# A sequence-mixing and MLP kernel: ScalarE issues the last piece's four stores of the first batch

## The chip, the cores and the metric

The kernel runs on one core of one Trainium2 chip. A core has TensorE (matmuls), VectorE, ScalarE, GpSimd and SyncE, and 16 DMA engines that all of them share. DMAs are issued from instruction queues, here from SyncE's and, for indirect ones, from GpSimd's. The metric is the device time of one execution in microseconds (us), lower is better.

## The reference

Three stages follow each other on x of shape (4, 4224, 192), batch by sequence by channels:

```python
# 1: causal convolution over the sequence, 7 taps per head, taps = softmax(weight), 8 heads of 24 channels
out = np.einsum('hk,bskhg->bshg', w, x_unf)
# 2: low-rank mixing over the sequence, then an MLP over the channels (192 -> 768 -> 192)
h = xt @ U @ V                        # U (4224, 32), V (32, 4224)
u = x + h.transpose(0, 2, 1)
x = u + np.maximum(u @ w_ch1, 0.0) @ w_ch2
# 3: real part of a 2D Fourier transform over sequence and channels, layer norm, an MLP
mixed = np.real(np.fft.fft(np.fft.fft(x, axis=1), axis=2))
u = x + mixed
un = (u - mean(u)) / np.sqrt(var(u) + 1e-06)
out = u + np.maximum(un @ w_ch1, 0.0) @ w_ch2
```

Stage 2 needs x @ U summed over the whole sequence of a batch (called t) before its first block can start. That is why the convolution of the first batch stands alone at the beginning.

## The kernel before

The program is written by hand, one instruction stream for each engine, with semaphores between them. fp32 operands are split in a high part and a low part in fp32r, and each product is made of several matmuls; hence the `..h`, `..l` and `..s` tiles.

**The opening.** The first batch is convolved in four pieces (`PIECES`, `NP` = 4) of 9, 9, 9 and 8 tiles of 122 rows, each in four pairs of heads (`PAIRS` = 4, so `FILLS` = 16 pairs in a batch). For each pair TensorE multiplies by the band matrix (line 910), ScalarE copies the result from the bank back into `xin0` (`first_convolved`, recorded as line 995, as all of ScalarE's copies are) and raises `act_x`. ScalarE and VectorE split the piece into `xhl`, and TensorE multiplies it by U (line 894) to add up t. After the last piece ScalarE copies the first V part (`v_high(0)`, `vch<-vraw`) and two pieces of the weights; VectorE makes their low parts and the sum of t (`tsb`, lines 1327 to 1331), both split it into `tst` (line 1355), and TensorE multiplies `tst` by V for the first block (`low_rank`, line 832).

**The convolved rows** go to HBM as well (`x_conv`), since the blocks of stage 2 read them in another layout. SyncE stores each piece (`store_x`) once its four pairs are copied: two stores of 112 and 10 rows (line 636), and for the last piece two more of 64 and 12 rows (line 640) for its last tile. When all stores of the batch have landed (`x_stored`, semaphores `x_out`, line 471), SyncE loads the first block into `ub` (`load_u`, line 659) and GpSimd the second, which is read backwards, with an indirect DMA (line 1498). VectorE adds the low-rank product to `ub` (line 1218 and 1221), TensorE transposes it (line 845), and the MLP begins (lines 792 to 815).

**The order on the queues.** SyncE's queue is in the order of the code: loads of x, U and V, the weights, the stores of the four pieces, the first `ub` load, the second weight of the MLP, the next batch's x, eight loads of V, then the stores and loads of V by way of `v_split`. V in split form goes out to HBM once and comes back block by block (`load_v`, lines 593 and 594), the first time for the third block.

**After the opening** 88 blocks of 384 rows follow (11 for each batch, and that twice, for stages 2 and 3). The convolution of later batches, the Fourier stages and the groups of spectrum rows are placed into numbered slots between the MLP matmuls.

Of the kernel before, what the change touches and what calls it, by code (L numbers as in the profile page):

```python
# [13 lines left out]
S, D, H, K, R = 4224, 192, 8, 7, 32  # L14
# [18 lines left out]
CT = N1 - PAD  # L33
NT = -(-S // CT)
TAIL = S - CT
OVER = (NT - 1) * CT - TAIL
PW = 9
PIECES = [(p, min(PW, NT - p)) for p in range(0, NT, PW)]
NP = len(PIECES)
PAIRS = H // 2  # L40
FILLS = NP * PAIRS
# [105 lines left out]
def program(nc, x, weight, U, V, w1a, w2a, w1b, w2b, f1, low, high, bc, mirror, backward_in, ident_in, out):  # L147
# [5 lines left out]
    xc = [hbm(f"x_conv{b}", (S, D)) for b in range(B)]  # L153
# [5 lines left out]
    with ExitStack() as ctx:  # L159
        def sb(name, shape, dt):  # L160
            return ctx.enter_context(nc.sbuf_tensor(name, shape, dt))

        def sem(name):
            return ctx.enter_context(nc.semaphore(name))
# [3 lines left out]
        with ExitStack() as early:  # L168
            xin0 = early.enter_context(nc.sbuf_tensor("xin0", [128, NT, D], F32))
# [5 lines left out]
        xin = [sb(f"xin{n + 1}", [128, PW, D], F32) for n in range(2)]  # L175
# [135 lines left out]
        for b in range(B):  # L311
            n0 = at[(0, b, 0)]
            for u in range(NB):
                w = b * NB + u
# [31 lines left out]
        for c in range(1, B):  # L346
# [13 lines left out]
            for k, (n, m) in enumerate(spots):  # L360
                p, first = k // 2, k % 2 * 2
# [67 lines left out]
        x_out = [sem(f"x_out{n}") for n in range(2)]  # L429
# [27 lines left out]
        def taken(e, key):  # L457

            q, k = fills[key]
            e.wait_ge(tb_free[q], k + 1)  # L460
# [3 lines left out]
        def pieces_out(c, p):  # L464

            return c * 64 + (p // 2 + 1) * 32 if p % 2 == 0 else c * 96 + (32 if p < NP - 1 else 96)

        def x_stored(e, c):

            e.wait_ge(x_out[0], pieces_out(c, NP - 2))  # L470
            e.wait_ge(x_out[1], pieces_out(c, NP - 1))

        def pair_of(c, p, k):

            return c * FILLS + p * PAIRS + k
# [72 lines left out]
        def _(e):  # L548
# [68 lines left out]
            def load_x(c, p):  # L617
                if c > 1 or p > 1:
                    before = (c, p - 2) if p > 1 else (c - 1, p + 2)
                    e.wait_ge(x_out[p % 2], pieces_out(*before))  # L620
                    e.wait_ge(pool_xl, pair_of(*before, PAIRS) - FILLS)
                j0, w = PIECES[p]
                e.dma_start(xin[p % 2][:, 0:w, :], x[c, :, j0:j0 + w, :]).then_inc(x_in[p % 2], 16)

            def store_x(c, p):
                j0, w = PIECES[p]
                src = xin0[0:CT, j0:j0 + w, :] if c == 0 else xin[p % 2][0:CT, 0:w, :]
                if c == 0:
                    e.wait_ge(act_x, pair_of(c, p, PAIRS))
                else:  # L630
                    taken(e, ("conv", c, p, PAIRS - 2))
                    taken(e, ("conv", c, p, PAIRS - 1))
                whole = w if p < NP - 1 else w - 1
                for a, z in ((0, 112), (112, CT)):
                    dst = bass.AP(xc[c].tensor, (j0 * CT + a) * D, [[D, z - a], [CT * D, whole], [1, D]])
                    e.dma_start(dst, src[a:z, 0:whole, :]).then_inc(x_out[p % 2], 16)
                if whole < w:
                    for a, z in ((OVER, OVER + 64), (OVER + 64, CT)):
                        dst = bass.AP(xc[c].tensor, (TAIL + a) * D, [[D, z - a], [1, D]])
                        e.dma_start(dst, src[a:z, whole, :]).then_inc(x_out[p % 2], 16)  # L640

            def rising(n, t):

# [7 lines left out]
            def load_u(n):  # L651
                if backward(n):
                    return
                ph, b, i = blocks[n]
                u_free(e, n)
                if i == 0:
                    x_stored(e, b)
                src, slot = rising(n, xc)
                e.dma_start(slot, src).then_inc(u_in[n % UR], 16)
# [44 lines left out]

            load_w1(0, w1a)
            store_x(0, 0)
            store_x(0, 1)
            store_x(0, 2)
            store_x(0, 3)
            load_u(0)  # L710
            load_w2(0, w2a)
            load_u(1)
# [58 lines left out]
            for t in range(TB):  # L771
                dst = bass.AP(out.tensor, b * (S * D) + (i * TB + t) * D, [[N2 * D, 128], [1, D]])
# [12 lines left out]
        def _(e):  # L785
# [92 lines left out]
            def part_of_t(c, p):  # L878
                j0, w = PIECES[p]
                if c == 0:  # L880
                    e.wait_ge(u_l, min(p + 1, len(U_PARTS)))
                    e.wait_ge(dve_xl, pair_of(0, p, PAIRS))
                    src = xhl if p % 2 == 0 else xhl1
                else:
                    e.wait_ge(pool_xl, pair_of(c, p, PAIRS) - FILLS)
                    src = xhl
                if c == 0:
                    q, first, last = 0, p == 0, p == NP - 1
                    o = tb[q]
                else:  # L890
                    o, q = empty(e, ("t", c, p))
                    first, last = True, True
                for j in range(w):
                    mm = e.matmul(o[0:2 * R, 0:2 * D], uhl[0:CT, j0 + j, :], src[0:CT, j].rearrange("p a d -> p (a d)"),  # L894
                                  start=(first and j == 0), stop=(last and j == w - 1))
                mm.then_inc(pe_tb[q] if last else pe_t0, 1)
# [96 lines left out]
        def _(e):  # L993
            def copy(o, i):
                return e.activation(o, i, ACT.Copy)  # L995
# [87 lines left out]
            def first_convolved(p, k):  # L1083
                f, j0 = pair_of(0, p, k), PIECES[p][0]
                bk = CONV_BANKS[f % len(CONV_BANKS)]
                e.wait_ge(pe_cv, f + 1)
                copy(tiles_of_pair(xin0[:, j0:], p, k), bank_of_pair(bk, p)).then_inc(act_x, 1)

            def first_high(p, k):
                wait(e, pe_t0, p - 1)  # L1090
                e.wait_ge(act_x, pair_of(0, p, k) + 1)
                copy(tiles_of_pair((xhl, xhl1)[p % 2][:, :, 0], p, k), tiles_of_pair(xin0[:, PIECES[p][0]:], p, k))\
                    .then_inc(act_xh, 1)

            def u_high(n):
                j = slice(*U_PARTS[n])
                e.wait_ge(ld_u, 16)
                copy(uhl[:, j, 0:R], u_raw[:, j]).then_inc(u_h, 1)
# [20 lines left out]
            def weights_high(n, part):  # L1119
                if part == 0:  # L1120
                    e.wait_ge(ld_w1[n], 48)
                    copy(w1h[n][:], w1l_raw[n][:]).then_inc(w_h[n], 1)
                elif part == 1:
                    copy(w1s[n][:], w1t_raw[n][:]).then_inc(w_h[n], 1)
                else:
                    e.wait_ge(ld_w2[n], 16)
                    copy(w2[n][:, :, 0:D], w2_raw[n][:, :, D:2 * D]).then_inc(w_h[n], 1)
# [3 lines left out]
            def v_high(n):  # L1131
                a, z = (v * 128 for v in V_PARTS[n])
                e.wait_ge(ld_v[n], 64)
                if n == 3:
                    e.wait_ge(v_stored[2], 16)
                copy(vpart[n], vraw[:, a:z]).then_inc(v_h, 1)

            for p in range(NP):
                for k in range(PAIRS):
                    first_convolved(p, k)  # L1140
                for k in range(0, PAIRS, 2):
                    first_high(p, k)
                if p < len(U_PARTS):
                    u_high(p)
            v_high(0)
            weights_high(0, 0)
            weights_high(0, 1)
# [425 lines left out]
```

## Time and profile before

| | |
|---|---|
| timed runs | 1247.24 us median of 3 (1245.2 to 1247.64) |
| the profiled execution | 1249.38 us, its span 1247.6 us |
| TensorE busy | 1217.3 us, 98% |
| VectorE busy | 829.9 us, 67% |
| ScalarE busy | 678.7 us, 54% |
| GpSimd busy | 424.3 us, 34% |
| SyncE's and GpSimd's queues | 133.95 MB and 18.99 MB |
| first transposes of TensorE (line 845) | from 37.47 us |

The span runs from the first to the last instruction of the profiled execution. Its own time is 1.8 us longer, and that execution is 2.1 us above the median of the timed ones. PE is TensorE, PEld its weight loads, DVE VectorE, ACT ScalarE, POOL GpSimd, SP SyncE; a q behind the name (SPq) is the engine's instruction queue, where DMAs are issued. L636 is line 636 of the kernel. An issue's duration is the time for which it held its queue; the data lands later.

### The profile page before, as it was taken

To read this page: it belongs to the slowest core of one execution; us is meant where nothing else is said; L and a number is where in the kernel's file an instruction comes from. 1 tells how busy PE (TensorE), PEld (TensorE's weight loads), DVE (VectorE), ACT (ScalarE), POOL (GpSimd) and SP (SyncE) were. 2 spreads that over 40 slices of the span, in tenths; PEclk is the share of its full clock that TensorE was granted. 3 is DMA by queue.
4 is the path that set the end of the run, shared out by engine and by line. 5 is a ranking of instruction groups with operands and counts; after the bars stand their busy time and mean duration, and the time that the engine had idled before them with its cause. 6 is when DMAs were issued, how large, how long until landed. Compare 5 with 4: busy or idle time off the path is not lost.

```text
span 1247.6 us, 23842 instructions
## 1 busy us (share of the span) xinstructions
PE 1217.3 (98%) x8404; PEld 1189.8 (95%) x8404; DVE 829.9 (67%) x2238; ACT 678.7 (54%) x1779; POOL 424.3 (34%) x541
## 2 busy tenths in 40 slices
PE   6899999999999999999999999999999999999998
PEld 5799999999998999999999999999999999999998
DVE  5565576777675577655556877765666777766564
ACT  5355555444566655445555666544445656655554
POOL 0133342343343245323333344521212344433331
PEclk9899999999999999999999999999999999999999
DMA  9867543344556533224434322322333233232221
GB/s 293 277 210 222 177 142 91 106 135 135 162 182 215 183 115 97 75 69 133 130 105 136 118 88 90 94 63 76 92 101 107 71 110 96 90 99 86 75 74 35
DMA packets 87967, 154.48 MB, mean 124 GB/s; under 512 B 11480, under 2 KB 47043, under 8 KB 87804
## 3 DMA queue, kind: packets, MB, share of 16 engines
q1 hardware_dynamic: 80232, 133.95, 34.0%
q0 software_dynamic: 7616, 18.99, 4.8%
q8 instruction: 68, 1.11, 0.4%
q14 instruction: 51, 0.42, 0.1%
HBM read 94.59 MB, written 63.32 MB: 127 GB/s over the span
## 4 chain that ended last, share of the span: by engine, by line
PE 93%; DMA 2%; DVE 2%; POOL 1%; SPq 1%; issue 1%; ACT 1%; ACTq 0%; POOLq 0%
PE bank L811 20%; PE bank L812 9%; PE bank L792 8%; PE bank L799 7%; PE bank L800 7%; PE bank L796 7%; PE bank L793 7%; PE bank L815 4%; PE bank L910 3%; PE bank L845 2%; PE bank L873 2%; PE bank L933 2%; PE bank L875 2%; PE bank L874 2%; PE bank L814 2%; PE bank L894 2%
## 5 line engine op out<-in xcount | busy, mean ns | idle before, releaser
L1005 ACT ACTIVATE ht<-bank 128x384 fp32r<-128x384 f32 x528 | 259.0, 491 | 472.0 <-PE bank L800 470.7
L1201 DVE SCALAR_TENSOR_TENSOR ht<-bank,ht 128x384 fp32r<-128x384 f32 x528 | 293.7, 557 | 332.7 <-ACT ht L1005 329.0
L811 PE MATMUL bank<-w,ht 128*128 128x384 f32 x1320 | 418.6, 366 | 0.8 <-DVE ub L1209 0.5
L812 PE MATMUL bank<-w,ht 128*128 128x192 f32 x1320 | 330.9, 251 | 0.0
L1460 POOL TENSOR_TENSOR ub<-ub,tmp 128x576 f32<-128x576 f32 x87 | 124.4, 1430 | 452.2 <-DVE ub L1209 310.6
L811 PEld LDWEIGHTS bank<-w,ht 128*128 128x128 f32 x1320 | 248.9, 189 | 3.9 <-issue 3.1
L812 PEld LDWEIGHTS bank<-w,ht 128*128 128x128 f32 x1320 | 252.4, 191 | 0.0
L792 PE MATMUL bank<-uth,w1h 128*128 128x384 f32 x528 | 189.4, 359 | 0.0
L799 PE MATMUL bank<-uts,w1s 128*128 128x384 f32 x528 | 179.0, 339 | 0.6 <-DVE uts L1234 0.6
L796 PE MATMUL bank<-utl,w1h 128*128 128x384 f32 x528 | 178.9, 339 | 0.5 <-DVE utl L1226 0.5
L793 PE MATMUL bank<-uth,w1l 128*128 128x384 f32 x528 | 178.8, 339 | 0.0
L800 PE MATMUL bank<-uts,w1t 128*128 128x384 f32 x528 | 178.2, 337 | 0.0
L1509 POOL DMA_INDIRECT mixed<-rowm,mir x84 | 82.7, 985 | 217.3 <-DVE rowm L1307 214.3
L793 PEld LDWEIGHTS bank<-uth,w1l 128*128 128x128 f32 x528 | 101.3, 192 | 0.0
L799 PEld LDWEIGHTS bank<-uts,w1s 128*128 128x128 f32 x528 | 99.5, 188 | 1.8 <-DVE uts L1234 1.4
L796 PEld LDWEIGHTS bank<-utl,w1h 128*128 128x128 f32 x528 | 99.8, 189 | 1.2 <-DVE utl L1226 1.2
L792 PEld LDWEIGHTS bank<-uth,w1h 128*128 128x128 f32 x528 | 100.1, 190 | 0.5 <-issue 0.5
L800 PEld LDWEIGHTS bank<-uts,w1t 128*128 128x128 f32 x528 | 99.5, 188 | 0.0
L815 PE MATMUL bank<-w,ht 128*128 128x384 f32 x264 | 81.9, 360 | 0.0
L1483 POOL TENSOR_TENSOR xhl<-xin,xhl 128x432 fp32r<-128x432 f32 (+1 forms) x48 | 52.4, 1113 | 82.3 <-ACT xhl L995 82.3
L873 PE MATMUL bank<-f1t,x2h 128*64 128x132 f32 (+1 forms) x264 | 62.6, 250 | 4.3 <-issue 3.7
L814 PE MATMUL bank<-w,ht 128*128 128x192 f32 x264 | 66.7, 253 | 0.0
(127 smaller groups left out, 2273.4 us busy)
## 6 DMA issues: line engine op xcount, KB each, us to landing
f1t<-f_copy SPq DMA_DIRECT2D x44, 396.0 KB, 3.3
ub<-x_two SPq DMA_DIRECT2D x44, 288.0 KB, 3.1
mix<-mixed SPq DMA_DIRECT2D x44, 288.0 KB, 3.3
out<-ub SPq DMA_DIRECT2D x43, 288.0 KB, 2.1
xin<-in_x SPq DMA_DIRECT2D x12, 864.0 KB, 7.1
x_conv<-xin SPq DMA_DIRECT2D x12, 756.0 KB
vch<-v_split SPq DMA_DIRECT2D x42, 192.0 KB, 2.8
mixed<-rowk SPq DMA_DIRECT2D x88, 74.2 KB
```

Of the source, the lines that this page charges most:

```text
L792: e.matmul(o, w1h[ph][:, c], uth[:, par], start=True, stop=False)
L793: e.matmul(o, w1l[ph][:, c], uth[:, par], start=False, stop=False)
L796: e.matmul(o, w1h[ph][:, c], utl[:, par], start=False, stop=False)
L799: e.matmul(o, w1s[ph][:, c], uts[:, par], start=False, stop=False)
L800: e.matmul(o, w1t[ph][:, c], uts[:, par], start=False, stop=True).then_inc(pe_up, 1)
L811: e.matmul(dn[t][:, 0:2 * D], hh, w2[ph][:, m, :], start=(m == 0), stop=False)
L812: mm = e.matmul(dn[t][:, 0:D], hl, w2[ph][:, m, 0:D], start=False, stop=False)
L814: e.matmul(dn[t][:, 0:D], hl, w2[ph][:, m, 0:D], start=False, stop=False)
L815: e.matmul(dn[t][:, 0:2 * D], hh, w2[ph][:, m, :], start=False, stop=True)\
L1005: e.activation(hth[q % 4], up[q % 3][:, 0:TOK], ACT.Relu).then_inc(act_h, 1)
L1201: e.scalar_tensor_tensor(htl[q % 4], up[q % 3][:, 0:TOK], 0.0, hth[q % 4].bitcast(F32), ALU.max, ALU.subtract).then_inc(dve_l, 1)
L1460: e.tensor_tensor(u_slot(n), u_slot(n), tmp[:], ALU.add).then_inc(pool_y, 1)
```

## The change

The stores of a piece become a function of their own, `piece_out`, that takes the engine which issues them. SyncE's `store_x` calls it after its wait, as before, for every piece but the last of the first batch. For that one ScalarE waits for `act_x` at 16 (all pairs copied) and calls `piece_out`, between its last `first_high` and `v_high(0)`. The semaphores that the stores raise, and the waits for them, are the same.

```diff
--- before.py
+++ after.py
@@ -470,6 +470,19 @@
             e.wait_ge(x_out[0], pieces_out(c, NP - 2))
             e.wait_ge(x_out[1], pieces_out(c, NP - 1))
 
+        def piece_out(e, c, p):
+
+            j0, w = PIECES[p]
+            src = xin0[0:CT, j0:j0 + w, :] if c == 0 else xin[p % 2][0:CT, 0:w, :]
+            whole = w if p < NP - 1 else w - 1
+            for a, z in ((0, 112), (112, CT)):
+                dst = bass.AP(xc[c].tensor, (j0 * CT + a) * D, [[D, z - a], [CT * D, whole], [1, D]])
+                e.dma_start(dst, src[a:z, 0:whole, :]).then_inc(x_out[p % 2], 16)
+            if whole < w:
+                for a, z in ((OVER, OVER + 64), (OVER + 64, CT)):
+                    dst = bass.AP(xc[c].tensor, (TAIL + a) * D, [[D, z - a], [1, D]])
+                    e.dma_start(dst, src[a:z, whole, :]).then_inc(x_out[p % 2], 16)
+
         def pair_of(c, p, k):
 
             return c * FILLS + p * PAIRS + k
@@ -623,21 +636,12 @@
                 e.dma_start(xin[p % 2][:, 0:w, :], x[c, :, j0:j0 + w, :]).then_inc(x_in[p % 2], 16)
 
             def store_x(c, p):
-                j0, w = PIECES[p]
-                src = xin0[0:CT, j0:j0 + w, :] if c == 0 else xin[p % 2][0:CT, 0:w, :]
                 if c == 0:
                     e.wait_ge(act_x, pair_of(c, p, PAIRS))
                 else:
                     taken(e, ("conv", c, p, PAIRS - 2))
                     taken(e, ("conv", c, p, PAIRS - 1))
-                whole = w if p < NP - 1 else w - 1
-                for a, z in ((0, 112), (112, CT)):
-                    dst = bass.AP(xc[c].tensor, (j0 * CT + a) * D, [[D, z - a], [CT * D, whole], [1, D]])
-                    e.dma_start(dst, src[a:z, 0:whole, :]).then_inc(x_out[p % 2], 16)
-                if whole < w:
-                    for a, z in ((OVER, OVER + 64), (OVER + 64, CT)):
-                        dst = bass.AP(xc[c].tensor, (TAIL + a) * D, [[D, z - a], [1, D]])
-                        e.dma_start(dst, src[a:z, whole, :]).then_inc(x_out[p % 2], 16)
+                piece_out(e, c, p)
 
             def rising(n, t):
 
@@ -706,7 +710,6 @@
             store_x(0, 0)
             store_x(0, 1)
             store_x(0, 2)
-            store_x(0, 3)
             load_u(0)
             load_w2(0, w2a)
             load_u(1)
@@ -1142,6 +1145,8 @@
                     first_high(p, k)
                 if p < len(U_PARTS):
                     u_high(p)
+            e.wait_ge(act_x, FILLS)
+            piece_out(e, 0, NP - 1)
             v_high(0)
             weights_high(0, 0)
             weights_high(0, 1)
```

On ScalarE, at the end of the opening, the order before was (`xin` and `xhl` are the last piece's copies, `vch` the first V part, `w1h` and `w1s` pieces of the first weight, `tst` the split sum t, `vmid` the second V part):

```order
L995 ACTIVATE xin<-bank 122x8x48 x4
L995 ACTIVATE xhl<-xin 122x8x48 x2
L995 ACTIVATE vch<-vraw 128x768
L995 ACTIVATE w1h<-w1l_raw 128x768
L995 ACTIVATE w1s<-w1t_raw 128x768
L995 ACTIVATE tst<-tsb 32x192 x2
L995 ACTIVATE vmid<-vraw 128x1152
```

and is now:

```order
L998 ACTIVATE xin<-bank 122x8x48 x4
L998 ACTIVATE xhl<-xin 122x8x48 x2
L480 DMA x_conv<-xin 112x7x192
L480 DMA x_conv<-xin 10x7x192
L484 DMA x_conv<-xin 64x192
L484 DMA x_conv<-xin 12x192
L998 ACTIVATE vch<-vraw 128x768
L998 ACTIVATE w1h<-w1l_raw 128x768
L998 ACTIVATE w1s<-w1t_raw 128x768
L998 ACTIVATE tst<-tsb 32x192 x2
L998 ACTIVATE vmid<-vraw 128x1152
```

Four DMA issues stand ahead of the first V copy and of all that ScalarE does later; nothing else has moved there.

On SyncE, from the third piece's stores, the order before was (`ub<-x_conv` is the first block's load, `w_raw` the second MLP weight):

```order
L636 DMA x_conv<-xin 112x9x192
L636 DMA x_conv<-xin 10x9x192
L636 DMA x_conv<-xin 112x7x192
L636 DMA x_conv<-xin 10x7x192
L640 DMA x_conv<-xin 64x192
L640 DMA x_conv<-xin 12x192
L659 DMA ub<-x_conv 128x576
L581 DMA w_raw<-in_moe_w_ch 128x6x192
```

and is now:

```order
L480 DMA x_conv<-xin 112x9x192
L480 DMA x_conv<-xin 10x9x192
L663 DMA ub<-x_conv 128x576
L594 DMA w_raw<-in_moe_w_ch 128x6x192
L636 DMA xin<-in_x 128x1728
```

The load of the first block follows the third piece's stores directly, behind its wait for all stores of the batch.

## Rows read from the trace of the kernel before

**Rows 1.** The page, part 1: busy us (share of span) xinstructions.
```profile
PE 1217.3 (98%) x8404; PEld 1189.8 (95%) x8404; DVE 829.9 (67%) x2238; ACT 678.7 (54%) x1779; POOL 424.3 (34%) x541
```

**Rows 2.** Waits of TensorE: waiting line, releaser: us in total, times, longest.
```profile
PE bank L845 <- DVE ub L1221: 3.3, 1, 3.3
...
PE bank L832 <- DMA vch<-v_split: 0.3, 1, 0.3
```

**Rows 3.** Chain of waits, 20 to 34.6 us: start, duration, what.
```profile
27.07 1.11 SPq L636
...
30.45 3.00 DMA x_conv<-xin
...
33.53 0.35 SPq L659
```

**Rows 4.** Windows: us, busy of PE, PEld, DVE, ACT, POOL, clock, DMA share, GB/s.
```profile
27.10:31.50 4.40, 2.31 (x13) 1.28 (x11) 4.23 (x9) 2.72 (x5) 0.00 (x0) 1.00 1.10 371
...
32.00:32.50 0.50, 0.00 (x0) 0.00 (x0) 0.22 (x1) 0.48 (x2) 0.00 (x0) 1.00 0.77 257
32.50:33.00 0.50, 0.00 (x0) 0.00 (x0) 0.47 (x2) 0.47 (x2) 0.00 (x0) 1.00 0.35 111
```

**Rows 5.** Timeline of SyncE's queue: start, duration to the last, issue, count.
```profile
30.45 1.02 SPq L640 DMA_DIRECT2D x_conv<-xin  x1
...
34.98 3.82 SPq L568 DMA_DIRECT2D vraw<-in_moe_V  x8
...
164.89 0.84 SPq L636 DMA_DIRECT2D x_conv<-xin  x2
165.78 2.36 SPq L640 DMA_DIRECT2D x_conv<-xin  x2
```

**Rows 6.** DMA queues from 164.4 to 165.4 us: packets, MB, share; q0 is GpSimd's.
```profile
q0 software_dynamic: 80, 0.29, 76.3%
```

**Rows 7.** Timeline of ScalarE: start, duration, out<-in, count.
```profile
26.31 0.49 ACT L995 ACTIVATE xin<-bank 122x384 f32<-122x384 f32 x1 [0.16 <-PE bank L910]
26.70 0.93 ACT L995 ACTIVATE xhl<-xin 122x384 fp32r<-122x384 f32 x2
27.52 0.83 ACT L995 ACTIVATE vch<-vraw 128x768 fp32r<-128x768 f32 x1
```

**Rows 8.** Timeline of VectorE: in brackets idle time before and who ended it.
```profile
28.76 0.95 DVE L1376 TENSOR_TENSOR vch<-vraw,vch 64x768 fp32r<-64x768 f32 x1
...
34.03 1.36 DVE L1376 TENSOR_TENSOR vmid<-vraw,vmid 64x1152 fp32r<-64x1152 f32 x1
36.54 0.56 DVE L1218 TENSOR_TENSOR ub<-bank,ub 128x384 f32<-128x384 f32 x1 [1.16 <-DMA ub<-x_conv]
```

**Rows 9.** Timeline of TensorE, 33 to 46 us.
```profile
33.26 0.93 PE L832 MATMUL bank<-tst,vch 128*128 128x192 f32 x3 [2.81 <-DVE tst L1355]
37.47 1.51 PE L845 MATMUL bank<-ident,ub 128*128 128x128 f32 x6 [3.28 <-DVE ub L1221]
...
41.26 0.52 PE L793 MATMUL bank<-uth,w1l 128*128 128x384 f32 x1
41.58 0.52 PE L796 MATMUL bank<-utl,w1h 128*128 128x384 f32 x1
...
45.23 0.33 PE L793 MATMUL bank<-uth,w1l 128*128 128x384 f32 x1
45.40 0.34 PE L796 MATMUL bank<-utl,w1h 128*128 128x384 f32 x1
```

**Rows 10.** Windows again: the third figure from the right is the granted clock.
```profile
33.30:43.50 10.20, 6.89 (x22) 5.81 (x23) 6.01 (x9) 3.46 (x6) 2.03 (x1) 0.50 0.90 264
...
402.00:405.30 3.30, 3.30 (x19) 3.30 (x19) 1.15 (x2) 1.16 (x2) 1.28 (x6) 0.50 0.93 294
```

**Rows 11.** Chain of waits, 33 to 60 us.
```profile
39.31 10.74 DMA v_split<-vmid
...
50.12 5.57 DMA vch<-v_split
```

## The prediction

> **What bounds the kernel now.** I read the page's busy times first: TensorE is busy for 98% of the span [rows 1], so a change counts only where it makes TensorE wait, or where it removes a wait. The waits of TensorE come next [rows 2]. The change touches one of the long ones: 3.3 us before the first transposes (line 845), put down to VectorE's line 1221, which is the first block's low-rank sum, written into `ub`. Later there is a short one, 0.3 us, on a tile of V that comes back from HBM.
>
> The chain of waits around it shows what the 3.3 us hang on [rows 3]: SyncE issues the four stores of the last piece from 27.07 us (two of line 636, two of line 640, the last at 30.45 us). The last store lands 3.00 us after that issue began, and only then, at 33.53 us, can SyncE issue the load of the first `ub` block. That load wakes VectorE at 36.54 us [rows 8], and TensorE's transposes start at 37.47 us [rows 9]. So what matters is when the last store *lands*. When it is issued matters only as far as it decides that.
>
> **What the change removes and adds.** SyncE loses four issues and the wait for `act_x` 16 in front of them. ScalarE gets them between its last `xhl` copies and its copy of the first V part, with all its later work behind them. I take the pieces in turn.
>
> *SyncE's side.* With the issues gone, SyncE comes to the wait for all stores at 27.1 us. Nothing is issued earlier on its queue, since `load_u(0)` is next and needs the landings. The gain here is what the landing gains.
>
> *The landing.* While SyncE issues those four stores, the DMA engines are busy without a break: share 1.10 from 27.1 to 31.5 us [rows 4]. The share falls to 0.77 in the half microsecond from 32.0 and to 0.35 in the next. So the stores are not late because they are issued late; they stand behind earlier transfers. Putting them in a second queue hands the same engines the same bytes. At most the uneven end could be filled: (1 - 0.77 + 1 - 0.35) x 0.5 us = 0.44 us. At least it gains 0. I take 0, the value nearest to the 1.10 row: the engines never starved ahead of the end.
>
> The Trainium skill says this outright ("DMA: Bandwidth & Descriptors", section "Issuing engines are not separate DMA queues"): whichever engine issues, the transfers run on the same 16 DMA engines, and issuing from several engines saves sequencer time alone. The trace agrees with its share of 1.10. By the same page's section "Why a DMA increments its semaphore by 16 and not by 1", a store of 10 or of 12 rows is spread over 10 or 12 engines, not 16. The uneven end would then be a matter of who owns which rows, and no queue would fill it, so by that rule the gain is 0 and not 0.44 us. The falling shares fit, but no row here names the engines.
>
> *ScalarE's side.* The trace has no DMA issue on ScalarE, so its price is bounded by SyncE's rows. Below: eight loads in a row took 3.82 us [rows 5], so 0.44 us each without the gaps, and four would take 4 x 0.44 + 3 x 0.04 = 1.9 us. Above: the same four stores, behind SyncE's backlog, took from 27.07 to 30.45 + 1.02 = 31.47 us, so 4.40 us [rows 3, 5]. Between them stands the nearest row. The last piece of the second batch is stored by four stores of the same shapes, with SyncE's queue empty before (from 164.4 to 165.4 us the only packets are those of GpSimd's queue [rows 6]). The first two took 0.84 us from 164.89 us and the other two 2.36 us from 165.78 us, so 165.78 + 2.36 - 164.89 = 3.25 us in all [rows 5]. The two small ones (64 and 12 rows) are the dear ones. SyncE seems to be held back until earlier descriptors have drained, even with nothing ahead of it in its queue. I take 3.25 us, as ScalarE's queue is empty too.
>
> The Trainium skill calls the sequencer time to start a DMA usually small beside the transfer (same page and section). By that, four issues would cost the 1.9 us of the loads. The row of 3.25 us differs, and I go by the row; the rule's result is rival A.
>
> When can the first issue start? Its wait (`act_x` 16) is met by the last `xin` copy, 26.31 + 0.49 = 26.80 us [rows 7]. The two `xhl` copies run until 27.6 us. If ScalarE's sequencer issues while they run, the start is about 26.88 us; if it waits for them, 27.67 us. I take the first: ScalarE starts instructions a little before the one ahead has ended (the copies at 26.31 us last until 26.80 us, the next begin at 26.70 us). The V copy then starts at 26.88 + 3.25 + 0.05 = 30.18 us where it started at 27.52 us. The delay of ScalarE is D = 2.7 us. With the later start D is 3.5 us; with 4.40 us of issues it is 3.8 us, and with both 4.6 us; with 1.9 us of issues, 1.3 us.
>
> *Who waits for ScalarE.* VectorE's split of that V part starts at 28.76 us, with no idle time before it, while the V copy ended at 27.52 + 0.83 = 28.35 us [rows 7, 8]. So the first 0.36 us of D (28.35 plus 0.05 us of handing over, to 28.76 us) cost nothing. The rest shifts the run of VectorE that follows: V part, W1, the sum of t, two pieces of `tst`, W1's tail, the second V part. It ends at 34.03 + 1.36 = 35.39 us, and the low-rank sum into `ub` is behind it in the same order. That sum starts at 36.54 us only because the DMA lands then; some 1.15 us are idle [rows 8]. So D is covered up to 0.36 + 1.15 = 1.51 us, and beyond it each microsecond delays TensorE's start by one. The other branch has more room: TensorE's low-rank product (line 832) ends at 33.26 + 0.93 = 34.19 us [rows 9], so 36.54 - 34.19 = 2.35 us beside the 0.36. With D = 2.7 us the cover is gone: TensorE starts late by L = 2.7 - 1.5 = 1.2 us. L is 2.0 us with the later start, 2.3 us with 4.40 us of issues, 3.1 us with both, and 0 with 1.9 us of issues.
>
> *What a late start costs in the end.* TensorE then works at half clock. Matmuls of 384 columns follow each other at 0.32 us (41.26, 41.58), and at 0.17 us (45.23, 45.40) once the granted clock has risen from 0.50 (1.2 GHz) to 1.00 (2.4 GHz) at 43.5 us, TensorE having been busy since 37.47 us [rows 9, 10]. If the clock rises at the same moment, a microsecond lost before it is worth 0.17/0.32 = 0.53 us; if it rises later with the start, a whole one. And TensorE meets a second gate at 55.74 us. A tile from `v_split` lands then (39.31 + 10.74, then 50.12 + 5.57 us, all of SyncE's own chain [rows 11]), and TensorE waits 0.3 us for it [rows 2]. That chain starts from the landing of the stores and not from ScalarE, so the first 0.3 us of lost TensorE time are given back. L = 1.2 us becomes 0.53 x 1.2 - 0.3 = 0.3 us to 1.2 - 0.3 = 0.9 us; I take the middle, 0.6 us.
>
> **Sum.** SyncE 0, landing 0, ScalarE's delay +0.6 us. The profiled execution took 1249.38 us (span 1247.6 and 1.8 us around it), and would take 1250.0 us. The median of the three timed runs is 1247.24 us, 2.1 us lower, and with the same 0.6 us it becomes 1247.8 us. That is 0.05%, and so no change that can be measured.
>
> **The rivals.**
>
> *A, the cover holds.* ScalarE's issues cost 0.44 us each as SyncE's loads do, D is 1.3 us, and nothing is late: +0.0 us, 1247.2 us. For it: an empty queue, and 1.3 lies under 1.51. Against: the 3.25 us of the same shapes from an idle queue.
>
> *B, the landing comes earlier.* The ragged end is filled, up to -0.44 us. VectorE's run then decides when the sum starts, so this needs A as well, and all 0.44 us only if D is below 1.07 us: 1246.8 us at best. For it: the shares 0.77 and 0.35. Against: the 1.10 ahead of them.
>
> *C, ScalarE is held back as SyncE was, and slower.* In this stretch the engines must also drain SyncE's backlog, so ScalarE's four issues take the 4.40 us of SyncE's. L is 2.3 to 3.1 us. It costs 0.53 x 2.3 - 0.3 = 0.9 us if the clock rises in place, and 3.1 - 0.3 = 2.8 us if it rises with the start. The rise can also slip: a short stretch at half clock lasts 3.3 us in this trace (402.0 to 405.3 us [rows 10]), and a rise that much later adds 0.47 x 3.3 = 1.6 us to the 0.9 us. So 1248.1 to 1250.0 us. It does harm from D = 1.51 us, and passes 0.2% from about L = 2.8 us with the clock against it. For it: SyncE's 1.02 us for a store of only 12 rows, in this very stretch. Against: ScalarE's own queue has nothing ahead in it.
>
> **Chances.** The forecast (L of 1 to 2 us) 45%, A 15%, B 5%, C 35%. What a measurement can tell from no change is about 0.2%, 2.5 us. Forecast, A and B lie inside it, and of C about a quarter may pass it: slower 9%. Faster by over 2.5 us has no mechanism here; the three timed executions lie 2.4 us apart, which leaves 4% for it. Same: 87%. The range takes B's end less the 2 us by which the lowest timed run lies under the median, 1244.9 us, and C's upper end, 1250.0 us.
>
> **What the profile after would show.** On ScalarE four issues, 3.2 us from the first to the last, from about 26.9 us, and the V copy from about 30.2 us; 1.9 us in all would be A, 4.4 us C. On SyncE the load of `ub` at 33.5 us again; 33.1 us would be B. VectorE's low-rank sum (line 1218) starts at 37.7 us, right behind the second V part and no longer behind the DMA, and the transposes at 38.7 us. TensorE's wait for `vch` near 55.7 us is gone, or the gate has moved. I am wrong if the landing moves by over 0.5 us, if VectorE's sum still waits for the DMA, or if a place after 60 us moves the end.

## The result

The changed kernel takes 1248.74 us, median of 22 runs (1246.35 to 1252.49). The kernel before takes 1246.5 us, median of 22 on the same chips (1245.13 to 1250.34). The ratio is 1.0016, 95% interval 1.0009 to 1.0024, so it is slower by 2.0 us, and by 1.1 to 3.0 us with the interval. That is clear of the noise, although the prediction called it a change that can't be measured; it had set that limit at about 2.5 us. It is more than the 0.6 us forecast, and lies within rival C (0.9 to 2.8 us). Run again as *e5* the changed kernel gave 1.0011 (1.0002 to 1.0020).

The page of its profiled execution (1246.96 us, one of the shorter ones):

```profile
span 1245.2 us, 23842 instructions
PE 1213.6 (97%) x8404; PEld 1186.2 (95%) x8404; DVE 829.2 (67%) x2238; ACT 678.9 (55%) x1779; POOL 423.7 (34%) x541
...
q1 hardware_dynamic: 79248, 133.24, 34.0%
q0 software_dynamic: 7616, 18.99, 4.7%
...
q10 hardware_dynamic: 984, 0.71, 0.2%
```

The new queue q10 holds the four stores, 984 packets that q1 no longer has. The span is 2.4 us shorter than in [rows 1]'s execution although the kernel is slower; that has to be cleared up first. [Rows 10] show a stretch at half clock at 402 us, and there is another at 521 us. The changed kernel's first profile has neither:

```profile
400.00:410.00 10.00, 8.95 (x66) 8.27 (x65) 5.47 (x18) 3.85 (x9) 3.72 (x7) 1.00 0.81 260
515.00:530.00 15.00, 13.39 (x99) 12.99 (x98) 9.45 (x31) 6.01 (x17) 4.83 (x5) 1.00 0.33 99
```

(windows; the clock is the third figure from the right: 1.00 in both). Such stretches come and go between executions of one kernel, so whole spans of single profiles can't be compared. A wait of TensorE just before does not tell them apart: near 518 us it waits 1.6 us in the changed kernel's first profile, where the clock stays up, and also in *e10*, a second profile of the kernel before, where the clock falls at 520 us. I compare a point instead that lies behind the opening and ahead of those stretches: the start of the 61st MLP activation on ScalarE. In the timelines of ScalarE it is at 184.85 us before

```profile
184.85 0.49 ACT L1005 ACTIVATE ht<-bank 128x384 fp32r<-128x384 f32 x1 [1.25 <-PE bank L800]
```

and at 186.32 us in the changed kernel:

```profile
186.32 0.49 ACT L1008 ACTIVATE ht<-bank 128x384 fp32r<-128x384 f32 x1 [1.25 <-PE bank L803]
```

From there to the end, profiles without such a stretch take 1058.5 us (*e11*), 1058.8 us (changed) and 1058.7 us (*e12*), those with one 1060.5 us (*e10*) and 1060.2 us (*e5*), and the kernel before with its two 1062.7 us. Each costs 1.5 to 2.0 us. So the loss that these profiles show is made in the opening: 1.5 us.

It is not shown that the change leaves such stretches alone. The timed executions list their mean granted clock. It is 0.9941 on average in 33 of the changed kernel and 0.9953 in the 93 of the kernel before for which it is on record, and 15 of the 33 but only 8 of the 93 are at 0.993 or lower. By my estimate that makes 0.0012 x 1247 / 0.5 = 3 us more at half clock. The openings profiled below show about 1 us of it: the half-clock part of the opening lasts 10.2 us in all three of the changed kernel, and 10.2, 6.8 and 10.2 us before. All three profiles of the changed kernel are of executions at 0.995 or 0.996, so where the rest lies is open. In time the opening suffices on average: the mean of those 33 is 1248.7 us, that of the 93 is 1247.2 us, 1.5 us apart.

In the opening the timeline of ScalarE shows the issues (ACTq) and what stands behind them:

```profile
26.77 0.49 ACT L998 ACTIVATE xin<-bank 122x384 f32<-122x384 f32 x1 [0.16 <-PE bank L913]
27.16 0.52 ACT L998 ACTIVATE xhl<-xin 122x384 fp32r<-122x384 f32 x1
27.29 0.38 ACTq L480 DMA_DIRECT2D x_conv<-xin  x1
27.57 0.51 ACT L998 ACTIVATE xhl<-xin 122x384 fp32r<-122x384 f32 x1
27.71 1.73 ACTq L480 DMA_DIRECT2D x_conv<-xin  x1
29.47 2.44 ACTq L484 DMA_DIRECT2D x_conv<-xin  x2
31.96 0.84 ACT L998 ACTIVATE vch<-vraw 128x768 fp32r<-128x768 f32 x1 [3.87 <-issue]
```

Only the first issue was cheap (0.38 us). The four held the queue from 27.29 to 31.91 us, 4.62 us in all, and the V copy started 5.19 us behind the last `xin` copy, where [rows 7] have 27.52 - 26.31 = 1.21 us. So D = 3.98 us. VectorE's timeline passes it on:

```profile
32.83 0.95 DVE L1381 TENSOR_TENSOR vch<-vraw,vch 64x768 fp32r<-64x768 f32 x1 [3.65 <-ACT vch L998]
...
38.10 1.35 DVE L1381 TENSOR_TENSOR vmid<-vraw,vmid 64x1152 fp32r<-64x1152 f32 x1
39.49 0.56 DVE L1223 TENSOR_TENSOR ub<-bank,ub 128x384 f32<-128x384 f32 x1
```

It now waits 3.65 us for ScalarE, and the low-rank sum follows the second V part without idle time. In [rows 8] it waited for the DMA. TensorE's timeline and SyncE's queue:

```profile
37.34 0.93 PE L835 MATMUL bank<-tst,vch 128*128 128x192 f32 x3 [6.42 <-DVE tst L1360]
40.41 1.51 PE L848 MATMUL bank<-ident,ub 128*128 128x128 f32 x6 [2.15 <-DVE ub L1226]
```

```profile
34.54 0.34 SPq L663 DMA_DIRECT2D ub<-x_conv  x1
```

The waits of TensorE in the opening were 2.8 and 3.3 us [rows 9] and are 6.4 and 2.1 us. The transposes start at 40.41 us and not at 37.47 us. The `ub` load was issued at 34.54 us, 1.0 us later than in [rows 3], but VectorE was not waiting for it.

### The profile page after: what moved, and what is told of

Its sections match the earlier page's. It is cut to its first block, busy times and chain, and to the rows that moved or that the text cites. A ratio compares the mean times of both kernels' runs of the same rounds, so it can differ in the third digit from the quotient of the medians.

```text
span 1245.2 us, 23842 instructions
## 1 busy us (share of the span) xinstructions
PE 1213.6 (97%) x8404; PEld 1186.2 (95%) x8404; DVE 829.2 (67%) x2238; ACT 678.9 (55%) x1779; POOL 423.7 (34%) x541
## 4 chain that ended last, share of the span: by engine, by line
PE 94%; DVE 2%; POOL 1%; issue 1%; ACT 1%; DMA 1%; ACTq 0%; DVEq 0%; POOLq 0%
PE bank L814 20%; PE bank L815 9%; PE bank L795 8%; PE bank L802 7%; PE bank L803 7%; PE bank L799 7%; PE bank L796 7%; PE bank L818 4%; PE bank L913 4%; PE bank L848 2%; PE bank L876 2%; PE bank L936 2%; PE bank L878 2%; PE bank L877 2%; PE bank L817 2%; PE bank L897 2%
```

## The experiments

One profile of each kernel is too few for differences of 1 us, so both kernels were profiled three times in all. All times below are from the profiles, in us of the span; V is the distance of the V copy from the last `xin` copy, start to start, and "clock up" the moment at which the granted clock went from 0.50 to 1.00 in the opening.

| kernel | V | `ub` load issued | transposes | clock up | 61st activation | ratio of times |
|---|---|---|---|---|---|---|
| before | 1.21 | 33.53 | 37.47 | 43.5 | 184.85 | 1 |
| e10, before again | 1.22 | 34.70 | 38.59 | 42.1 | 185.40 | 0.9994 (0.9984 to 1.0003) |
| e11, before, third | 1.22 | 34.10 | 37.92 | 42.9 | 184.70 | |
| changed | 5.19 | 34.54 | 40.41 | 44.5 | 186.32 | 1.0016 (1.0009 to 1.0024) |
| e5, changed again | 4.02 | 34.17 | 40.11 | 46.0 | 186.82 | 1.0011 (1.0002 to 1.0020) |
| e12, changed, third | 5.14 | 34.24 | 40.11 | 43.8 | 186.06 | |
| e1, delay alone | 5.19 | 34.20 | 40.34 | 44.0 | 186.19 | 1.0007 (0.9998 to 1.0017) |
| e7, short delay | 2.44 | 33.81 | 38.36 | 42.2 | 185.23 | 1.0006 (0.9996 to 1.0015) |
| e9, double delay | 8.95 | 34.84 | 44.61 | 48.7 | 190.40 | 1.0043 (1.0029 to 1.0057) |
| e2, GpSimd issues | 1.22 | 34.19 | 38.44 | 42.0 | 185.63 | 1.0004 (0.9995 to 1.0013) |
| e4, one of four | 1.21 | 34.37 | 38.32 | 44.0 | 186.43 | 1.0010 (1.0001 to 1.0020) |
| e8, behind copies | 1.21 | 34.65 | 38.48 | 42.9 | 185.52 | 1.0003 (0.9992 to 1.0013) |
| e3, VectorE's order | 5.44 | 35.20 | 39.15 | 43.2 | 186.29 | 0.9999 (0.9990 to 1.0008) |
| e6, w1 behind stores | 1.22 | 31.74 | 36.76 | 40.3 | 183.41 | 0.9987 (0.9978 to 0.9996) |

**e10 and e11, the kernel before, unaltered.**

> The kernel before, unaltered, for a second profile. Its opening is to show how much of the difference is scatter: the 61st MLP activation starts at 184.9 us of the span in its first profile, at 186.3 and 186.8 us in the two of the changed kernel. Theory: 184.5 to 185.6 us here, the ub load issued at 33.5 to 33.9 us, a wait for that load of about 1 us on VectorE. If it comes at 186 us or later, the openings differ by chance and the loss is not placed yet.

> The kernel before a third time, for its profile: as for the second, 184.5 to 185.6 us at the 61st activation and the ub load issued at 33.5 to 33.9 us. With the two delay kernels these make five profiles with all stores on SyncE; the theory that ScalarE's queue also makes the landing later wants them below 34.2 us, where the profiles with ScalarE issuing lie at 34.2 to 35.2 us.

The 61st activation came where it was expected (185.40, 184.70 us). The expectation on the `ub` load was missed: 34.70 and 34.10 us, with all stores on SyncE. So nothing shows that ScalarE's queue makes the stores land later: the six profiles with all stores on SyncE and the old order of loads (the three of the kernel before, *e1*, *e7* and *e9*) have that load at 33.53 to 34.84 us, and the three of the changed kernel at 34.17 to 34.54 us. The mean of the 61st activation in the three profiles of the kernel before is 184.98 us, and their scatter 0.7 us. A kernel timed against itself came out at 0.9994, so 0.0006 in one timing of this size says nothing.

**e5 and e12, the changed kernel, unaltered.**

> The changed kernel once more, unaltered, for a second profile and more times. In its first profile it is 1.0 us behind the kernel before at the 61st MLP activation, counted from the last copy into xin, though TensorE started 2.5 us late; its median was 2.2 us above. Theory: ratio 1.0010 to 1.0022 again, L near 2.5 us again, and the time from L to the end varies with the moment at which the clock rises: 0.9 us if it rises as early as in the first profile, 2.2 to 2.5 us if it rises later with the start. Rival 2 (stretches at half clock later on made the median): ratio back within 1.0008 with the same opening.

> The changed kernel a third time, for its profile. Theory: ScalarE's four issues take 3.4 to 4.7 us, VectorE's sum starts behind the second V part and not behind the DMA, TensorE's transposes start at 40 us or later, the ub load is issued at 34.2 us or later and the 61st activation starts at 186 to 187 us.

The 61st activation is at 186.06 to 186.82 us, mean 186.40 us, and the two kernels' values don't overlap: 1.4 us. The means of the transposes' starts are 37.99 and 40.21 us, so L = 2.2 us. The issues took 3.43 us in *e5* and 4.57 us in *e12*. *e5* shows why L does not follow: its last `xin` copy came late (27.64 us), so the V copy still started at 31.66 us.

The hold has an end rather than a length. The first issue begins anywhere from 26.74 us (*e3*) to 28.17 us (*e5*), but the last one ends between 31.59 and 31.91 us in all five profiles in which ScalarE issues all four. SyncE's own last store issue ended at 31.26 to 31.94 us in the three profiles before. In *e6*, below, with fewer bytes ahead, it ends at 29.80 us.

The ratio of *e5*, 1.0011, is in the range expected, and of the three it has the latest rise of the clock (46.0 us) with the latest 61st activation. Rival 2, the stretches, would have it back within 1.0008. That is below the 1.0011 but inside its interval, so this timing does not exclude it.

**e1, e7, e9: the delay without the DMAs.** ScalarE copies something that nothing reads; the stores stay on SyncE.

```diff
+            e.wait_ge(ld_w1[0], 48)
+            for g in range(4):
+                copy(ht[:, g * F:(g + 1) * F], w1l_raw[0][:])
+            copy(w1h[1][:], w1l_raw[0][:])
+            copy(w1s[1][:, 0:256], w1l_raw[0][:, 0:256])
             v_high(0)
```

(*e7*: one such copy and one of 480 elements; *e9*: eleven.)

> The stores stay on SyncE as before; ScalarE makes six copies that nothing reads, ahead of the first V copy, for about 4.0 us (5 x 0.73 + 0.3), as long as the changed kernel's V copy was late. Theory (the loss is ScalarE's lateness, handed on by VectorE): VectorE's low-rank sum starts near 39 us, behind the second V part and not behind the DMA, the first ub load is issued at 33.5 us, and the time is 1 to 2.5 us above before, ratio 1.0008 to 1.0020. Rival 1 (the second DMA queue, or the later landing that the changed kernel showed, costs the time): ratio 1.0000, within 0.5 us. Rival 2 (the half-clock stretches later on decide, whatever the opening does): ratio within 0.0005 of 1 and stretches at random places.

> As the delay alone, but with two copies (about 1.2 us), under the cover of 1.5 us that the prediction read from VectorE. Theory: VectorE's low-rank sum still waits for the DMA, its idle time falls from 1.16 us to 0.3 us, and at the 61st MLP activation the run is within 0.3 us of the kernel before: no loss. Rival (ScalarE's delay counts from its first microsecond): 0.5 us or more behind there.

> As the delay alone, but ScalarE makes eleven copies, for about 7.7 us, ahead of the first V copy, so L is near 6.2 us. What a microsecond of late start is worth: if the clock's rise moves with TensorE's start, the time is 6.2 - 0.3 = 5.9 us above before, ratio 1.0047; if the rise stayed in its place and lost time counted 0.53, 3.0 us, ratio 1.0024. The first is expected now, since the changed kernel lost about 2 us for L of 1.5 to 2.5 us.

*e1* is the changed kernel's opening without any second queue. ScalarE and VectorE in its timelines:

```profile
31.90 0.83 ACT L995 ACTIVATE vch<-vraw 128x768 fp32r<-128x768 f32 x1
```

```profile
32.76 0.95 DVE L1381 TENSOR_TENSOR vch<-vraw,vch 64x768 fp32r<-64x768 f32 x1 [3.63 <-ACT vch L995]
...
39.42 0.56 DVE L1223 TENSOR_TENSOR ub<-bank,ub 128x384 f32<-128x384 f32 x1
```

V copy at 31.90 us and sum at 39.42 us, against 31.96 and 39.49 us; 61st activation at 186.19 against 186.32 us. So in the profile ScalarE's lateness alone makes the whole loss. The `ub` load, expected at 33.5 us, was at 34.20 us, as late as in the changed kernel. The time (1.0007) is just short of the range expected, and its interval reaches from below 1 to beyond the changed kernel's ratio, so the timing alone decides nothing.

*e7*: with D = 2.44 - 1.21 = 1.2 us the 61st activation is 0.25 us behind the mean of the kernel before, inside its scatter. VectorE had no idle time left ahead of the sum, where it was expected to wait 0.3 us for the DMA:

```profile
37.44 0.56 DVE L1221 TENSOR_TENSOR ub<-bank,ub 128x384 f32<-128x384 f32 x1
```

Its ratio (0.9996 to 1.0015) fits no loss and a loss of 0.5 us alike. The cover is no fixed 1.5 us: VectorE's idle time ahead of the sum is 1.16 us in [rows 8] and, in *e10* and *e11*,

```profile
37.66 0.56 DVE L1218 TENSOR_TENSOR ub<-bank,ub 128x384 f32<-128x384 f32 x1 [1.33 <-DMA ub<-x_conv]
```

```profile
36.99 0.56 DVE L1218 TENSOR_TENSOR ub<-bank,ub 128x384 f32<-128x384 f32 x1 [0.21 <-DMA ub<-x_conv]
```

so with the free 0.36 us it is 0.6 to 1.7 us.

*e9* prices a late start: L = 44.61 - 37.99 = 6.6 us, and the time is up by 0.0043 x 1247.1 = 5.4 us (3.6 to 7.1 us). The 61st activation is 5.4 us later too. That is 0.8 us for each microsecond, or (5.4 + 0.3) / 6.6 = 0.87 with the gate's 0.3 us added back. The 3.0 us expected of a rise that stays in place (3.2 us with L = 6.6 us) lies outside the interval, and the rise did move: to 48.7 us.

**e2: GpSimd issues the four stores**, ahead of its first indirect load; ScalarE issues nothing (the stores get a semaphore of their own).

```diff
+            e.wait_ge(act_x, FILLS)
+            piece_out(e, 0, NP - 1, [x_pool])
             e.wait_ge(ld_back, 16)
             load_falling(1)
```

> GpSimd issues the last piece's four stores, ahead of its first indirect load, where it only waits otherwise; ScalarE issues nothing. Theory: ScalarE's V copy is back at 27.5 us and VectorE's run ends near 35.4 us, so the time is that of before, ratio 0.9997 to 1.0005, if the landing stays within 0.5 us; each microsecond by which GpSimd's issues make the landing later costs 0.5 to 1 us. Rival 1 (stores in a second queue interleave with SyncE's and land later): the first ub load is issued at 34.1 us or later, and the loss of 1.0016 stays.

```profile
28.17 1.74 POOL L485 DMA_DIRECT2D x_conv<-xin  x2 [25.63 <-ACT xin L1003]
29.89 1.11 POOL L489 DMA_DIRECT2D x_conv<-xin  x2
```

(GpSimd's timeline; in brackets the idle time it had before.) The issues took 2.8 us of an engine that would have waited anyway. The `ub` load was issued at 34.19 us, the transposes at 38.44 us lie in the range of the kernel before, and no loss can be measured (1.0004, at most 1.0013). So the loss of 1.0016 did not stay, although the stores went through a second queue. The 61st activation is 0.2 us beyond the latest of the kernel before, though; *e4* shows where such a loss can come from. The landing criterion of rival 1 (34.1 us or later) was met, but *e10* and *e11* meet it too with one queue, so it tells nothing.

**e4: ScalarE issues one store of the four**, SyncE the other three.

```diff
             e.wait_ge(act_x, FILLS)
-            piece_out(e, 0, NP - 1)
+            piece_out(e, 0, NP - 1, (0,))
```

> ScalarE issues only the first of the four stores (112 rows); SyncE issues the other three. Theory: that first issue took 0.38 us in the changed kernel and the holding back only began with the second, so ScalarE's V copy is late by 0.4 us or less, the cover of 1.5 us holds, and the ratio is 0.9997 to 1.0004. Rival 1 (two queues interleave; 784 of the 930 rows of data are still in the second one): the landing is still 0.5 us later and most of the loss of 1.0016 stays.

ScalarE was not late at all (V 1.21 us), and the transposes started at 38.32 us. Yet the 61st activation was at 186.43 us and the ratio 1.0010. This is against the theory. TensorE's waits from 50 to 62 us show where the profile lost it:

```profile
PE bank L837 <- DMA vch<-v_split: 1.2, 1, 1.2
```

That is the second gate: the tile's load was issued at 52.30 us, against 50.12, 50.77 and 50.37 us in the kernel before. The V store ahead of it was issued at 41.33 us (39.31 to 40.64 us before) and took 10.9 us (10.7 and 10.1 us in two of those). The clock's rise at 44.0 us was late as well.

The same wait stands in the other two kernels in which another engine issues stores and the V copy is not late. These are the rows of *e2* and of *e8*, from 50 to 62 us:

```profile
PE bank L840 <- DMA vch<-v_split: 1.0, 1, 1.0
```

```profile
PE bank L835 <- DMA vch<-v_split: 0.8, 1, 0.8
```

The kernel before has 0.3, 0.6 and 0 us there, but *e7*, with all stores on SyncE, has 0.7 us. The three kernels are at 185.5 to 186.4 us at the 61st activation, each a little beyond the 184.7 to 185.4 us of the kernel before. So a second queue may cost up to about 1 us by way of this gate (an estimate: 1.2 us in *e4* less the 0.3 us of the kernel before). No run isolates that, and why the V store lands late is open. Rival 1, as far as it says that most of the loss stays, is not excluded by *e4*'s own ratio; against it stand *e1*, with the loss and one queue, and *e8*, below. The changed kernel loses nothing at this gate, for its TensorE comes later.

**e8: ScalarE issues all four, behind its copies** of the V part and of two weight pieces.

```diff
-            e.wait_ge(act_x, FILLS)
-            piece_out(e, 0, NP - 1)
             v_high(0)
             weights_high(0, 0)
             weights_high(0, 1)
+            e.wait_ge(act_x, FILLS)
+            piece_out(e, 0, NP - 1)
```

> ScalarE issues the four stores behind its copies of the V part and of the two weight pieces, where it waited 2.0 us for VectorE's tsb in the kernel before. Theory: the first issue comes near 29.8 us, and if the four still take 3 to 4.6 us they end at 33 to 34.4 us, so ScalarE is late only from tst on, by 1.3 to 2.6 us; the last store lands 1 to 2 us later than in the changed kernel, since its data is now asked for late, and the sum starts behind the DMA at 38 to 39 us: about as slow as the changed kernel. Rival (only the time on ScalarE counts): VectorE's run ends 1.3 us earlier than in the changed kernel and most of the loss is gone.

The theory had the issues begin near 29.8 us, behind the copies, and delay `tst`. The timeline of ScalarE shows otherwise:

```profile
28.14 0.38 ACTq L480 DMA_DIRECT2D x_conv<-xin  x1
28.42 0.52 ACT L998 ACTIVATE xhl<-xin 122x384 fp32r<-122x384 f32 x1
28.55 1.07 ACTq L480 DMA_DIRECT2D x_conv<-xin  x1
28.83 0.83 ACT L998 ACTIVATE vch<-vraw 128x768 fp32r<-128x768 f32 x1
29.57 0.83 ACT L998 ACTIVATE w1h<-w1l_raw 128x768 fp32r<-128x768 f32 x1
29.66 1.49 ACTq L484 DMA_DIRECT2D x_conv<-xin  x1
30.30 0.83 ACT L998 ACTIVATE w1s<-w1t_raw 128x768 fp32r<-128x768 f32 x1
31.18 0.56 ACTq L484 DMA_DIRECT2D x_conv<-xin  x1
```

The issues begin 0.52 us behind the start of the last `xin` copy, just as in the changed kernel, although three copies stand ahead of them. They then run *beside* these copies: 3.6 us of issues (28.14 to 31.74 us), and the V copy is not late. So the copies that stand ahead had been handed on to the engine before the issues began, and only what stands *behind* the issues is held. The Trainium skill ("Advanced Engine Details and Errata", section "Engine Queue Depths") gives ScalarE's queue a depth of 8 instructions. The five copies that overlap the issues here fit in that, and no run shows the depth itself. The rival came out, and more: VectorE's run ends at 36.68 us, 2.8 us earlier than in the changed kernel. The last store does not land 1 to 2 us later, since the `ub` load is at 34.65 us. The same four issues, moved by three lines, cost 1.0003 (0.9992 to 1.0013) and not 1.0016 or 1.0011. This is the plainest evidence that their time counts only where work waits behind them.

**e3: VectorE's order.** The changed kernel, with the low-rank sum ahead of W1's tail and the second V part.

```diff
             t_low(0)
-            weights_low(1)
-            v_low(1)
...
                     make_u(n)
+                    weights_low(1)
                     turned_low(n)
+                    v_low(1)
                     weights_low(2)
```

> The changed kernel, ScalarE still issuing, but VectorE makes the first block's low-rank sum ahead of W1's tail and of the second V part, which follow it. Theory: the sum needs only tst and the DMA, so it starts near 37.5 us and not 39.5 us; TensorE's transposes start near 38.4 us, W1's tail is done in time for the first MLP matmuls or holds them by under 0.5 us, and 1 to 1.5 us of the loss come back: ratio 1.0000 to 1.0008. Rival 1 (queue or landing): ratio stays 1.0016. Rival 2 (clock stretches): stays 1.0016 with stretches that this does not move.

```profile
36.06 0.74 DVE L1360 TENSOR_TENSOR tst<-tsb,tst 32x192 fp32r<-32x192 f32 x2 [0.56 <-ACT tst L998]
38.23 0.56 DVE L1223 TENSOR_TENSOR ub<-bank,ub 128x384 f32<-128x384 f32 x1 [1.42 <-DMA ub<-x_conv]
```

VectorE is free from 36.8 us and waits for the DMA again, with ScalarE as late as ever (V 5.44 us). The transposes start 1.1 us earlier than in the changed kernel's mean. The 61st activation (186.29 us) is only 0.1 us earlier, for the new order has a price of its own. TensorE now waits for the low part of the second MLP weight, which VectorE makes behind the second V part, and for the `v_split` tile. The waits of TensorE from 40 to 62 us, where the changed kernel has neither:

```profile
PE bank L795 <- DVE w L1387: 0.6, 1, 0.6
PE bank L835 <- DMA vch<-v_split: 0.2, 1, 0.2
```

The timed runs do show a gain (0.9999; the interval ends at 1.0008, below the changed kernel's first, which begins at 1.0009, and not below its second, which begins at 1.0002). So the sum's start hangs on VectorE's order as the theory said, and what that is worth is open between 0.1 and 2 us.

**e6: the first MLP weight behind the stores.** The one thing that [rows 4] call for: fewer bytes ahead of the stores. SyncE, ScalarE and VectorE do their part of that weight later; the stores stay on SyncE.

```diff
-            load_w1(0, w1a)
             store_x(0, 0)
...
             store_x(0, 3)
+            load_w1(0, w1a)
             load_u(0)
```

> The kernel before, with SyncE's three loads of the first MLP weight moved behind the stores of the four pieces and ahead of the first ub load, and the copies and low parts of that weight on ScalarE and VectorE moved behind the V parts and, on VectorE, behind the low-rank sum. 768 KB no longer stand ahead of the stores. Theory (the landing of the stores is bound by the transfers ahead of it): at some 370 GB/s they land 2 us earlier, the ub load is issued near 31.5 us, the low-rank sum starts near 34.9 us and the first MLP matmul near 37.8 us and not 39.0 us: 0.6 to 1.5 us gained, ratio 0.9988 to 0.9996. Rival (the landing hangs on when the issues are made): the ub load is issued near 33.5 us still and nothing is gained, or VectorE's new order loses up to 1 us.

```profile
27.03 0.82 SPq L636 DMA_DIRECT2D x_conv<-xin  x2
27.89 1.91 SPq L640 DMA_DIRECT2D x_conv<-xin  x2
29.84 0.36 SPq L576 DMA_DIRECT2D w1l_raw<-in_moe_w_ch  x1
30.25 1.17 SPq L578 DMA_DIRECT2D w1t_raw<-in_moe_w_ch  x2
31.74 0.34 SPq L659 DMA_DIRECT2D ub<-x_conv  x1
```

The first of the four stores was issued at 27.03 us, as in [rows 3] (27.07 us). The last issue ended at 29.80 us, where it ended at 31.26 to 31.94 us before, so it was held for less time. The `ub` load, which follows the landing, is 2.4 us earlier than the mean before (34.11 us). So the bytes ahead bind both the issues and the landing. The sum started at 35.84 us and not 34.9 us: the `ub` load took 4.1 us from its issue to the sum, against 2.9 to 3.0 us before, probably because the weight now goes ahead of it. The time is 0.9987, 1.6 us less (0.5 to 2.7 us): this version beats both kernels. The edit also changes VectorE's order as *e3* does, and no run separates the two.

## Why the forecast came out too small

The mechanism came out as forecast: ScalarE's lateness goes through VectorE's run to TensorE, and the sum waits no longer for the DMA. The size did not: 2.0 and 1.4 us in the two timings, not 0.6 us. The measured time lies inside the range because that reached up to rival C's end. "No change that can be measured" held only for so coarse a limit: 22 runs of each kernel do show the change.

- *SyncE's side and the landing: 0.* Right. The `ub` load is at 34.17 to 34.54 us against 33.53 to 34.70 us before, and *e6* shows what would move it.
- *Start of the issues: 0.57 us behind the last `xin` copy's start.* Right: 0.52 us.
- *Price of four issues: 3.25 us.* This is the term that was mis-sized: 4.62, 3.43 and 4.57 us, on average 1.0 us more. I had taken a store pattern behind an empty queue. ScalarE's queue was empty too, but SyncE's earlier stores were still being transferred, so 4.40 us, SyncE's own price in this very stretch, was the nearer row. Rival C named it. Nearer still would have been the moment at which SyncE's row ends, 31.47 us: the V copies start at 31.64 to 31.96 us. The first issue on ScalarE took 0.36 to 0.38 us in every profile, and the later ones waited.
- *The cover: 1.51 us.* Right in kind (*e1*, *e7*), but one profile gave one value of something that moves between 0.6 and 1.7 us.
- *L: 1.2 us.* Measured 2.2 us; the 1.0 us more is that of the issues.
- *Price of a late start: between 0.53 and 1 us for a microsecond, less the gate's 0.3 us.* The upper end was nearer. The clock's rise moves with TensorE's start: its mean went from 42.8 to 44.8 us, by 1.9 us, where the start went by 2.2 us. *e9* gives 0.87 us ahead of the gate, and the middle that was taken is 0.77 us. With L = 2.2 us the one makes 2.2 x 0.87 - 0.3 = 1.6 us and the other 1.4 us, beside 1.4 us at the 61st activation and 2.0 and 1.4 us in the two timings. So this term added little to the miss.
- *The gate's 0.3 us.* Right for the changed kernel: its wait is gone from the list. But the gate is no constant: 0.3, 0.6 and 0 us in the kernel before, and up to 1.2 us in *e4*.

Rival A and rival B are out: no cover held, and no landing came earlier. Rival C's mechanism is what happened, without a slip of the clock's rise in the three profiles. Whether there is one in the executions with a lower clock is not known.

## What to carry to other kernels

A DMA issue on a compute engine's queue costs what stands behind it, not what already runs beside it: put it behind the next few instructions of that engine, or on an engine that waits anyway. Take its price from a row in the same stretch with the DMA engines equally loaded, and look at the moment when the hold ends rather than at its length: here it ended near 31.7 us whenever the issues began, though they had a queue of their own. When a load waits for stores to land and the DMA engines are full, look at the bytes ahead of the stores, not at who issues them.

## What was not expected

- Four stores held ScalarE's queue for 3.4 to 4.9 us (4.9 us in *e3*), the first of them for only 0.38 us. GpSimd's four took 2.8 us (*e2*).
- ScalarE's issues ran beside three of its copies (*e8*).
- The same kernel has none, one or two stretches at half clock behind 400 us (3.4 us each), worth 1.5 to 2.0 us apiece. A single execution can't show a change of 2 us beside them.
- Low mean clocks are more frequent in the changed kernel's executions (15 of 33 against 8 of 93), and no profile shows why.
